# Remainder rows in whole lines, next weights prepared first, and the six-tile expert first, in a gated recurrence with a mixture of experts

## The reference, cut to what matters

```python
p = domain_probs / (domain_probs.sum(-1, keepdims=True) + 1e-09)   # [1536, 4]
for e in range(4):                       # w1[e]: 320 x 1024, w2[e]: 1024 x 320
    h = np.maximum(x @ w1[e], 0.0)
    out += p[:, e:e + 1] * (h @ w2[e])
```

## Time and profile before

| | us |
|---|---|
| median of three runs | 428.01 (427.45 to 428.79) |
| the profiled execution | 427.77 |
| its span, first to last instruction | 426.0 |
| TensorE matmuls busy in the span | 406.7 (95%) |
| VectorE busy | 272.1 (64%) |
| POOL busy | 219.2 (51%) |
| ScalarE busy | 192.5 (45%) |
| mean granted clock of TensorE | 0.984 of full speed |

### The profile page before, as it was taken

How to read it: one execution, slowest core, us unless ns; L and a number is a source line. 1 busy time by engine, 2 the same in 40 slices (tenths; PEclk the granted TensorE clock), 3 DMA queues, 4 the chain that set the end, 5 groups by cost and what they waited for, 6 DMA issues and landing times.

```text
span 426.0 us, 7291 instructions
## 1 busy us (share of the span) xinstructions
PE 406.7 (95%) x2650; PEld 390.4 (92%) x2650; DVE 272.1 (64%) x483; ACT 192.5 (45%) x378; POOL 219.2 (51%) x233
## 2 busy tenths in 40 slices
PE   8999999998999999999999399988999999999997
PEld 8889999997999999999999399877999999999997
DVE  6866795856545448355255372657787778887763
ACT  5475476857252657324122333354443543444420
POOL 5855744669731759604000961664467545676400
PEclk9999999998999999999999699999999999999999
DMA  8899949657850505305024001202220122212002
GB/s 273 257 302 378 341 134 352 230 204 287 282 203 0 219 5 214 121 1 208 0 49 103 13 2 69 93 1 82 81 80 10 72 82 80 76 30 89 0 2 92
DMA packets 20933, 54.49 MB, mean 128 GB/s; under 512 B 2369, under 2 KB 12114, under 8 KB 19746
## 3 DMA queue, kind: packets, MB, share of 16 engines
q1 hardware_dynamic: 20322, 52.63, 35.7%
q10 hardware_dynamic: 576, 1.40, 1.0%
HBM read 50.40 MB, written 2.05 MB: 123 GB/s over the span
## 4 chain that ended last, share of the span: by engine, by line
PE 84%; SPq 4%; DVE 3%; issue 3%; ACT 2%; DMA 2%; POOL 2%; DVEq 0%; ACTq 0%; POOLq 0%
PE acc_ps L1599 18%; PE hid_ps L1580 17%; PE acc_ps L1663 15%; PE out_ps L1536 5%; SPq L509 3%; PE hid_ps L1663 3%; PE out_ps L1639 2%; PE out_ps L1641 2%; PE acc_ps L1580 2%; PE out_ps L1642 2%; PE out_ps L1640 2%; PE out_ps L1543 2%; PE score_ps L1480 2%; PE score_ps L1639 1%; PE add_ps L1515 1%
## 5 line engine op out<-in xcount | busy, mean ns | idle before, releaser
L1167 DVE SCALAR_TENSOR_TENSOR h_lo<-hid_ps,h_hi 128x384 fp32r<-128x384 f32 (+1 forms) x70 | 36.0, 514 | 100.0 <-ACT h_hi L835 99.8
L835 ACT ACTIVATE h_hi<-hid_ps 128x384 fp32r<-128x384 f32 (+1 forms) x70 | 31.8, 455 | 110.1 <-PE hid_ps L1580 110.0
L1599 PE MATMUL acc_ps<-w_hi,h_hi 128*128 128x320 f32 x208 | 67.3, 323 | 8.2 <-DVE h_lo L1167 7.4
L1599 PE MATMUL acc_ps<-w_hi,h_lo 128*128 128x320 f32 x208 | 64.9, 312 | 0.0
L1599 PE MATMUL acc_ps<-w_lo,h_hi 128*128 128x320 f32 x208 | 64.7, 311 | 0.0
L611 POOL TENSOR_TENSOR w_lo<-w_raw,w_hi 128x384 fp32r<-128x384 f32 x40 | 47.7, 1196 | 22.3 <-ACT w_hi L821 22.3
L1580 PE MATMUL hid_ps<-xt_hi,w_hi 128*128 128x384 f32 (+1 forms) x210 | 57.7, 329 | 0.3 <-ACT w_hi L821 0.3
L1580 PE MATMUL hid_ps<-xt_hi,w_lo 128*128 128x384 f32 (+1 forms) x210 | 57.2, 327 | 0.6 <-POOL w_lo L611 0.6
L1599 PEld LDWEIGHTS acc_ps<-w_hi,h_hi 128*128 128x128 f32 x208 | 40.0, 192 | 9.4 <-DVE h_lo L1167 7.7
L585 POOL TENSOR_SCALAR_AFFINE_SELECT dec_w<-dec_w 128x512 f32<-128x512 f32 x22 | 16.3, 742 | 53.2 <-ACT dec_w L800 53.1
L1599 PEld LDWEIGHTS acc_ps<-w_lo,h_hi 128*128 128x128 f32 x208 | 40.0, 192 | 0.1
(11 more groups left out here) (255 smaller groups left out, 1034.7 us busy)
## 6 DMA issues: line engine op xcount, KB each, us to landing
w_raw<-in_w_b SPq DMA_DIRECT2D x19, 704.0 KB, 7.8
w_raw<-in_w_s SPq DMA_DIRECT2D x12, 832.0 KB, 4.4
raw<-in_qk_s SPq DMA_DIRECT2D x8, 1024.0 KB
g_all<-g_dram SPq DMA_DIRECT2D x10, 512.0 KB, 7.8
kv<-in_kv_n SPq DMA_DIRECT2D x12, 352.0 KB, 6.7
q_pack<-in_q_p SPq DMA_DIRECT2D x10, 192.0 KB, 7.5
out_y<-y_acc SPq DMA_DIRECT2D x12, 160.0 KB, 1.8
carry<-g_dram SPq DMA_DIRECT2D x30, 60.0 KB
```

The source lines that it names most:

```text
L835: nc.scalar.activation(h_hi[:, M % RING, 0:cols], hid_bank(M)[:, 0:cols], ACT.Relu).then_inc(hid_hi, 1)
L1167: nc.vector.scalar_tensor_tensor(h_lo[:, M % RING, 0:cols], hid_bank(M)[:, 0:cols], 0.0, h_hi[:, M % RING, 0:cols].bitcast(fp32), ALU.max, ...
L1599: last = nc.tensor.matmul(acc_ps[t][:, 0:DM], x, w, start=(f == 0 and i == 0), stop=(f == NF - 1 and i == 2))
```

## The change

Four things are done, and with them the matching waits and counts.

1. **Remainder rows in whole lines.** rest_hi and rest_lo become [96, 2, 1024]: for each k the eight tiles of a row stand as they do in xt_hi. 12 copies of 128 KB (pieces of 4 KB) take the place of 24, each k with a semaphore of its own. POOL adds k = 0 and makes the first difference, then k = 1 and the other three. The readers of one half now step through it in pieces of 128.
2. **Operands' rounding in other slots.** See the table in the diff; product 1 of step 0 goes into slot 72.
3. **Next step's weights first.** own_highs(2), sums_highs(2), step_sums(2), sums_lows(2) and step_rest_low(2) are done in or right after slots 78 and 79; later steps do them early in the step; wide_low for 22 comes last.
4. **The expert with six tiles first**: EXPERTS (2, 1, 0), FIRST_PAIR (1, 0, 0).

```diff
-SUB = {... 6: (26, 28), ...}
+SUB = {... 6: (26, 27), ...}
-EXPERTS = (1, 0, 2)
-FIRST_PAIR = (0, 0, 1)
-BEGIN = 73
+EXPERTS = (2, 1, 0)
+FIRST_PAIR = (1, 0, 0)
+BEGIN = 72
-        rest_hi, rest_lo = between("rest_hi", [REM, 4, WIDE]), between("rest_lo", [REM, 4, WIDE])
+        rest_hi, rest_lo = between("rest_hi", [REM, 2, 2 * WIDE]), between("rest_lo", [REM, 2, 2 * WIDE])
@@ load_rest (SP)
-                for part, raised, lowered in ((rest_hi, 64, 96), (rest_lo, 0, 32)):
-                    for k, first in enumerate((raised, lowered)):
-                        source = halves(xt_hi[first:first + 32, 2, :].bitcast(fp32))
+                for k in range(2):
+                    for part, first in ((rest_hi, 64), (rest_lo, 0)):
+                        source = xt_hi[first + 32 * k:first + 32 * (k + 1), 2, FIRST_WIDE * L:NT * L].bitcast(fp32)
                         for r in range(3):
-                            for half in range(2):
-                                ...
+                            sp.dma_start(part[32 * r:32 * (r + 1), k, :], source).then_inc(rest_in[k], 16)
@@ rest_whole, turn_rest (POOL)
-                pool.wait_ge(rest_in, 24 * 16)
+                pool.wait_ge(rest_in[k], 6 * 16)
+                nc.gpsimd.tensor_tensor(rest_hi[:, k, :], rest_hi[:, k, :], rest_lo[:, k, :], ALU.add).then_inc(rest_ready, 1)
...
+                if which == 1:
+                    pool.wait_ge(rest_ready, 1)
+                    nc.gpsimd.tensor_tensor(t_1, j_1, i_1, ALU.subtract).then_inc(rest_t_ready, 1)
+                    return
...
@@ slots of POOL
-64 step_sums(0); 65 rest_whole(0), rest_whole(2); 66 own_lows(0); 67 turn_rest(); 70 step_sums(1); 74 own_lows(1); 78 add_22(0)
+64 step_sums(0); 65 own_lows(0), rest_whole(0), turn_rest(1); 66 rest_whole(1), turn_rest(2); 69 step_sums(1); 71 own_lows(1); 77 add_22(0); 78 step_sums(2)
@@ steps t of POOL
-step_sums(t+1), own_lows(t+1), step_down_low(t+1), add_22(t)
+own_lows(t+1), step_down_low(t+1), add_22(t), step_sums(t+2)
@@ slots of ScalarE (each after the slot's relu)
-65 own_highs(0); 66 sums_highs(0); 68 round_rest(0, 3); 69 round_t(0), round_t(2); 71 round_rest(3, 2), round_rest(5, 2); 73 own_highs(1); 74 keep_1(0), sums_highs(1); 75 step_down_high(0); 76 keep_5(0)
+65 own_highs(0), sums_highs(0); 67 round_t(0), round_t(2); 69 round_rest(0), own_highs(1); 70 round_rest(1); 71 sums_highs(1); 73 keep_1(0); 75 step_down_high(0), keep_5(0); 79 wide_relu(0, 21), own_highs(2), sums_highs(2)
@@ steps t of ScalarE
-keep_1, own_highs(t+1), keep_5, step_down_high(t+1), sums_highs(t+1), relu 11, 22, 21, 12
+own_highs(t+1), keep_1, sums_highs(t+1), step_down_high(t+1), keep_5, relu 11, 21, 12, 22
@@ slots of VectorE (each after the slot's hidden_low)
-64 make_whole(0); 65 make_whole(1); 66 turn_whole(0); 67 turn_whole(1), sums_lows(0); 68 step_rest_low(0); 69 rest_lows(0, 3, 0); 70, 71 t_lows; 72 rest_lows(3, 2, 1), rest_lows(5, 2, 2); 75 add_2(0); 76 sums_lows(1); 77 add_3(0), step_rest_low(1); 78 wide_low 11; 79 add_21(0)
+64 make_whole(0); 65 make_whole(1), turn_whole(0); 66 turn_whole(1), sums_lows(0); 67 step_rest_low(0); 68, 69 t_lows; 70 rest_lows(0) in three pieces; 71 rest_lows(1); 72 sums_lows(1); 73 step_rest_low(1); 74 add_2(0); 76 add_3(0); 78 wide_low 11, add_21(0); 79 wide_low 21, add_12(0), then add_expert(9)
+sums_lows(2), step_rest_low(2) ahead of wide_low(0, 12) and wide_low(0, 22)
@@ steps t of VectorE
-add_wide 0, add_2, add_wide 1, 2, add_3, add_wide 3, sums_lows(t+1), low 11, add_21, step_rest_low(t+1), low 22, low 21, add_12, low 12
+add_wide 0, add_2, sums_lows(t+1), step_rest_low(t+1), add_wide 1, 2, add_3, add_wide 3, low 11, add_21, low 21, add_12, low 12, low 22
@@ product (TensorE)
-                        pe.wait_ge(rest_low, 3)
+                        pe.wait_ge(rest_low, 2)
```

More of the change, by code:

```diff
@@ L332, in build @@
         down_done, acc_ready, acc_free = sem("down_done"), sem("acc_ready"), sem("acc_free")
-        rest_in, whole_ready, rest_ready = sem("rest_in"), sem("whole_ready"), sem("rest_ready")
+        rest_in, whole_ready, rest_ready = [sem(f"rest_in{i}") for i in range(2)], sem("whole_ready"), sem("rest_ready")
         t_ready, rest_t_ready, t_high, t_low = sem("t_ready"), sem("rest_t_ready"), sem("t_high"), sem("t_low")
@@ L741, in _ @@
                 if M == 65:
+                    own_lows(0)
                     rest_whole(0)
-                    rest_whole(2)
+                    turn_rest(1)
                 if M == 66:
[L745 to L748, removed]
+                    rest_whole(1)
+                    turn_rest(2)
+                if M == 69:
                     step_sums(1)
-                if M == 74:
+                if M == 71:
                     own_lows(1)
@@ L763, in _ @@
                 add_22(t)
+                if t + 2 < STEPS:
+                    step_sums(t + 2)
         @block.scalar
@@ L1266, in t_lows, with rest_lows @@
                                         t_hi[:, first:first + 2, :].bitcast(fp32), ALU.subtract).then_inc(t_low, 1)
-            def rest_lows(first, n, at):
-                dve.wait_ge(rest_high, at + 1)
-                source = rest_hi[64:REM, 0:3, :] if first == 0 else rest_t[64:REM, first - 3:first - 3 + n, :]
-                low = rest[64:REM, first:first + n, :]
-                nc.vector.tensor_tensor(low, source, low.bitcast(fp32), ALU.subtract).then_inc(rest_low, 1)
+            def rest_lows(which):
+                if which == 0:
+                    dve.wait_ge(rest_high, 2)
+                    for k, half, at in ((0, 0, 0), (1, 0, 1), (1, 1, 2)):
+                        low = rest[64:REM, at, :].rearrange("p (i l) -> p i l", l=L)
+                        last = nc.vector.tensor_tensor(low, halved(rest_hi[64:REM, k, :])[:, half], low.bitcast(fp32), ALU.subtract)
+                else:
+                    dve.wait_ge(rest_high, 3)
+                    low = rest[64:REM, 3:7, :]
+                    last = nc.vector.tensor_tensor(low, rest_t[64:REM], low.bitcast(fp32), ALU.subtract)
+                last.then_inc(rest_low, 1)
             def sums_lows(q):
@@ L1338, in _ @@
                     hidden_low(ahead)
+                if M == 79:
+                    wide_low(0, 21)
+                    add_12(0)
                 if M == 0:
@@ L1411, in _ @@
                 wide_low(t, 12)
+                wide_low(t, 22)
             for t in range(STEPS, STEPS + 2):
```

137 lines of the change are left out of this document (70 added, 67 removed).

## The result

| | before | changed | ratio, 95% interval |
|---|---|---|---|
| first measurement, median of 4 | 428.40 us (427.45 to 429.24) | 423.97 us (422.22 to 425.53) | 0.9896 (0.985 to 0.9943) |
| again, beside experiment 11, 11 and 6 executions | 428.11 us | 423.57 us (422.05 to 424.49) | 0.9892 (0.9861 to 0.9923) |
| profiled execution: time, span | 427.77, 426.0 us | 424.52, 422.8 us | |
| mean granted clock in it | 0.984 | 0.992 | |

The change gains 4.5 us. The forecast was 424.5, its range 416.5 to 427.0. The sum came out right, but by luck in part: two terms that the prediction does not have, a gain of 2.4 us and a loss of about 3, nearly cancel.

What follows compares the result with a forecast made beforehand. TensorE, busy 95%, was taken as the bound, so gains come only from its stops, chiefly 7.4 us behind late remainder rows. Gains 1.8 + 0.7 + 0.9 = 3.4 us from 428.0 gave 424.6, said as 424.5; range 416.5 to 427.0.

Steps and rivals of the forecast that it cites:

- before product 1 of step 0: Stage ahead of step 0's first wide product: loss falls from 10.2 to 8.4 us, gain 1.8.
- steps after it: Waits in steps 1 and 2 after step 0's first product: 2.6 us for 3.3, gain 0.7.
- 10.2: Loss before product 1 in the old kernel: 7.4 us standing, 2.6 of half clock, 0.2 for the last L1273.
- Part 1: Remainder-row copies on SP: 12 whole-line copies, issued by 224.6 and landed by 226.7 us instead of 234.6.
- the walk: VectorE and POOL instruction by instruction from 222 us: TensorE loses 1.6, 3.3, 0.7 and 0.9, together 6.6 us.
- Part 2: Remainder work before product 1: POOL and VectorE exclude each other for whole instructions, costing 6.6 us before any clock fall.
- the slower rival: POOL's turns of the remainder rows: pieces of 128 elements double them, giving 429.0 to 429.5 us; chance 0.06.
- in later steps ... TensorE covers it: Later steps: swapped ScalarE, VectorE and POOL instructions cost nothing; were cover to fail, 10 us.
- the second fall of the clock: At slot 72 or in step 1: another clock fall costs 2.5 us, giving 427.0; chance 0.09.
- The clock before product 1: After the 3.3 us stop: half speed costs 2.5 us less 0.7 hidden at slot 72, so 1.8.
- the clock holds: Rival at the 3.3 us stop: exclusion but no clock fall, 1.8 us less, 422.7 us; chance 0.22.
- Part 4: Last expert, with the six-tile expert moved first: the short breaks near the end go, gain 0.9 us.

Runs made afterwards that it cites:

- experiment 11: Experiment 8's kernel with sums_lows(0) and the turns a slot earlier or later and own_lows(0) behind POOL's turns: 414.16 us, ratio 0.9682 to the kernel before.
- experiment 4: Changed kernel with POOL's two additions and four turns of the remainder rows cut to one column each: 416.91 us, ratio 0.9741 to the kernel before.
- experiment 1: Kernel before with only unit 6's second subtract moved from slot 28 to 27: 426.01 against 428.22 us, ratio 0.9957.
- experiment 8: Changed kernel, same instructions reordered: product 1 in slot 73, VectorE's remainder work spread between h_lo, later evictions ahead of step_rest_low: 417.51 us, ratio 0.9772.
- experiment 10: Experiment 8's kernel with the expert order of before (EXPERTS 1, 0, 2): 417.60 us, ratio 0.9768 to the kernel before.
- experiment 12: The changed kernel itself, rerun on the chip of experiment 11: 423.57 us, ratio 0.9892 to the kernel before.
- experiment 3: Changed kernel with unit 6's second subtract put back from slot 27 to 28: 425.27 us, ratio 0.9937 to the kernel before.
- experiment 6: Experiment 5's kernel plus the expert with six tiles first, other orders as before: 422.89 us, ratio 0.9847 to the kernel before.
- experiment 2: Kernel before with only the remainder rows fetched in 12 whole-line copies, everything in its old slot: 421.64 us, ratio 0.9853.
- experiment 5: Kernel before with the whole-line copies and unit 6's subtract in slot 27, nothing else: 421.25 us, ratio 0.9818.

## Why the prediction was right, and where it was not

| | predicted gain | in the profile |
|---|---|---|
| slot 27 (early stage) | none named | 2.4 |
| before product 1 of step 0 | 1.8 | 2.3 |
| steps after it | 0.7 | -2.4 |
| the end | 0.9 | 0.9 |
| sum | 3.4 | 3.2 (426.0 - 422.8) |

The second row is 10.2 less 7.9. Down 67 could start at 223.68 (226.05 less 2.37) and starts at 225.37, 1.7 late; down 68 is another 3.4 late (231.53 for 228.09), product 1 another 2.8 (246.53 for 243.72). The third row is what closes the account: between product 1 and the last matmul, the slot taken off, the changed kernel is 1.5 us slower, the end's 0.9 included. The rows bear it out. By the starts of matmuls its waits in step 1 and 2 are 0.7, 1.15 and 0.8, together the 2.65 that the prediction's terms add up to; to them come 1.7 for the second fall and 0.8 and 0.6 at 289 and 300.

That the sum fits is luck. Without the 2.4 of slot 27, which the forecast does not have, and with all its other terms as measured, it would have been 0.8 for 3.4.

**Hit.** The copies are over by 225, as Part 1 has it, with some luck: eleven issues of 0.6 us and one of 1.8 take 8.8 us, not 7.8, but SP starts 2.37 earlier for the subtract's sake. Once these 2.37 are added, each end in the walk, from own_lows to L1299, comes within 0.2 us of its row. The exclusion of Part 2 is shown, by experiment 4 against the changed kernel and not only by rows 7: without POOL's part the same order of VectorE has no stop. That bears out what the Trainium skill says in "SBUF — State Buffer", section "Who interferes with whom". The walk gave 1.6, 3.3 and 0.9 for rows of 1.53, 3.16 and 0.98, and the waits of step 1 and 2 came as 0.52, 0.99 and 0.60 in the rows, which count from modelled ends, for 0.5, 1.15 and 0.8. The break-free end came too. No stride made POOL's turns slower: L679 takes 1.29 at 232.10, the L670 of before took 1.27, so the slower rival had no ground.

**The step that failed first** is an omission: the diff's SUB edit has no term. It is worth 2.4 us in the rows, 1.8 (0.7 to 3.0) by the ratio of experiment 1. No row that the prediction uses is from before 193 us; the wait of 2.10 at 98.84 has no part in it.

**The second** is "in later steps ... TensorE covers it", argued from busy shares in 300:320. Two waits of 0.67 and 0.46 came in the steps of three pairs, behind an L1308 of 2.47. The busy share of VectorE there is no answer to which instruction stands ahead of the evictions. Experiments 8 and 10 remove both by order alone.

**The third** is the second fall of the clock, priced 2.5 and given 0.09 as a case of its own. In this profile it came, in step 1, at two thirds of the price: 3.4 us at half speed are 1.7. It does not come each time. Experiment 12's profile of the same kernel has the same stops of 0.53 and 0.99 there and a clock of 1.00 in 274:275; its second fall is at 11:15, in a part that the change leaves alone. The time goes with the number of falls; where they lie is known for the two profiled executions alone. Over both measurements the changed kernel took 422.0 to 423.6 us with a mean clock of 0.996 (five executions), 423.6 to 424.5 with 0.992 (four) and 425.5 with 0.988 (one), and one fall is 0.004. So the rival of two falls was no rival to the forecast but a part of its scatter.

**The clock before product 1** was the right event at the wrong price. The forecast took 1.8 net of 2.5 less 0.7; experiment 3 shows 0.13 net (15.00 against 14.87 us), because VectorE's queue ends last at product 1 and swallows it. The same holds for the "2.6 of half clock" in the 10.2 us of before. In experiment 1 half speed lasts 3.1 us behind the stop of 7.4 instead of 5.3, and yet product 1 starts 12.10 us after the down that ends the stop (239.62 to 251.72), for 12.19 before: TensorE waits 0.93 there, until VectorE is through. So 2.2 us less of half speed, 1.1 us of work, brought product 1 forward by 0.1: that much of the 2.6 was no price of the clock. The forecast and the rival "the clock holds" were the same time in these executions.

**Part 4** was right in its row; its cause is not borne out. The breaks go with the orders of the later steps alone (experiment 10, with the orders of experiment 8), and the six tiles first alone bring new ones (experiment 6).

That the whole change was worth less than its first part was open to the prediction's own walk and not asked: it showed that the turn moved up one slot delays down 67 by 1.6, and took that as a price without working out the old slots beside it.

## What to carry to other kernels

Where two engines take turns at a port, ask of each instruction that may meet the other what is queued behind it and who waits for that. The sum of the work sets less than the place of the urgent item: the same instructions took 423.6 us in one order and 414.2 in another. Price each edit of a change alone, the smallest number in a table too, and against the edit left out.

## What was not expected of the hardware

- Whether a stop lets the clock fall is not settled by its length. A stop of 3.16 us was followed by a fall (the changed kernel), one of 3.19 was not (experiment 3); one of 2.62 was (experiment 8, granted clock 0.50 in 234:236), one of 2.64 was not (experiment 2). Shorter ones differ too: one of 1.38 left it at 1.00 before, one of 1.39 in experiment 5 was followed by 0.65 in 282:283 and 0.50 in 283:284. In experiment 12 it fell to 0.53 in 11:12 though TensorE had stood nowhere for 0.2 us in 6:11. What decides is open.
- With no stop over 1 us behind the start the scatter goes too: experiment 4's six executions lie within 0.8 us, the 20 of the kernel before beside them within 5.4.
- "Whoever waited goes next" holds for most meetings, not for all. L1308 asks at 231.51 while POOL's L677 runs to 232.14; POOL's L679 goes first, and L1308 ends at 234.34, 0.95 after it. In experiment 4 it asks at 225.88 and three sums of POOL pass it (225.93, 226.62, 227.32), 3.13 us for 1.08. Which one passes was not tried.
- A copy of 128 KB in whole lines costs SP 0.59 us to issue (median), one of 64 KB in short pieces 0.60: here twice the bytes cost nothing at issue. One of the twelve took 1.84, as one of the 24 took 1.27.
